# A fused attention, expert and feed-forward kernel: load order at the start, the links of routing, and a first chunk in two banks

## The reference

```
q_bits = (einsum('bhsd,dk->bhsk', q, proj) > 0); same for k
scores = where(q_bucket == k_bucket, scale * q @ k.T, -1e9)
attn   = exp(scores - max) / (sum + 1e-9);  x = attn @ v
```

```
logits = x @ w_gate + modality_bias[modality_id];  e = argmax(logits)
out[e_idx == e] = gate * (relu(x @ w1[e]) @ w2[e])         # 512 -> 1024 -> 512
h = x @ w_in;  g = max(h, 0) + alpha * min(h, 0);  y = g @ w_out   # 512 -> 2048 -> 512
```

## Time and profile before

| | before |
|---|---|
| median of 3 runs | 696.58 us (695.50 to 698.93) |
| profiled execution | 695.9 us, span 694.0 us |
| busy PE, PEld | 684.2, 610.8 us |
| busy DVE, ACT, POOL | 465.9, 353.9, 223.3 us |
| granted TensorE clock | 1.00 |

### The profile page before, as it was taken

How to read it: one execution, slowest core, us unless ns; L and a number is a source line. 1 busy time by engine, 2 the same in 40 slices (tenths; PEclk the granted TensorE clock), 3 DMA queues, 4 the chain that set the end, 5 groups by cost and what they waited for, 6 DMA issues and landing times.

```text
span 694.0 us, 12262 instructions
## 1 busy us (share of the span) xinstructions
PE 684.2 (99%) x4049; PEld 610.8 (88%) x4051; DVE 465.9 (67%) x1017; ACT 353.9 (51%) x692; POOL 223.3 (32%) x320
## 2 busy tenths in 40 slices
PE   7999999999999999999999999999999999999998
PEld 5899999999999998889988998888888888888886
DVE  6998989899999989523511216666676666666664
ACT  5888888888887783114311215333343333433332
POOL 8855465555657960412014200600017000010000
PEclk9999999999999999999999999999999999999999
DMA  6995766749363513870113008200003000010001
GB/s 180 214 263 158 202 206 152 221 117 253 94 168 90 197 40 104 295 248 30 45 60 95 26 31 274 60 0 0 0 16 106 0 0 0 1 60 0 0 1 60
DMA packets 48243, 70.58 MB, mean 102 GB/s; under 512 B 7294, under 2 KB 27470, under 8 KB 48198
## 3 DMA queue, kind: packets, MB, share of 16 engines
q1 hardware_dynamic: 41636, 57.50, 29.0%
q0 software_dynamic: 2832, 8.45, 4.1%
q10 hardware_dynamic: 3730, 4.07, 1.7%
HBM read 33.46 MB, written 17.30 MB: 73 GB/s over the span
## 4 chain that ended last, share of the span: by engine, by line
PE 87%; DVE 6%; ACT 2%; DMA 2%; POOL 1%; issue 1%; SPq 1%; ACTq 0%; DVEq 0%; POOLq 0%
PE bank L1005 7%; PE bank L1232 6%; PE bank L1222 6%; PE bank L1223 6%; PE bank L1233 6%; PE bank L1234 6%; PE bank L1224 6%; PE bank L1024 4%; PE bank L989 4%; PE bank L1026 4%; PE bank L990 4%; PE bank L1167 3%; PE bank L1171 3%; PE bank L1169 3%; PE bank L1130 3%; PE bank L1131 3%
## 5 line engine op out<-in xcount | busy, mean ns | idle before, releaser
L1337 ACT ACTIVATE probs<-bank,raffine 128x768 f32<-128x768 f32 x96 | 95.3, 992 | 28.7 <-DVE raffine L1624 28.4
L1616 DVE TENSOR_REDUCE bank<-bank 128x1 f32<-128x768 f32 x96 | 92.2, 961 | 4.7 <-PE bank L990 3.6
L1005 PE MATMUL bank<-cst,probs 128*128 128x128 f32 x576 | 80.4, 274 | 1.0 <-DVE pt_lo L1632 0.3
L1481 ACT ACTIVATE wi_hi<-ff_raw 128x512 fp32r (+1 forms) x48 | 30.4, 633 | 90.9 <-PE bank L1224 90.8
L1925 DVE SCALAR_TENSOR_TENSOR ht_lo<-bank,ht_hi 128x512 fp32r<-128x512 f32 x28 | 19.0, 689 | 85.4 <-ACT ht_hi L1423 85.4
L1005 PEld LDWEIGHTS bank<-cst,probs 128*128 128x128 f32 x576 | 67.3, 140 | 9.0 <-issue 3.9
L1632 DVE TENSOR_TENSOR pt_lo<-bank,pt_hi 128x384 fp32r<-128x384 f32 x128 | 70.5, 551 | 6.0 <-ACT pt_hi L1354 3.8
L1222 PE MATMUL bank<-x_hi,wi_hi 128*128 128x512 f32 (+1 forms) x192 | 74.5, 388 | 0.0
L1223 PE MATMUL bank<-x_lo,wi_hi 128*128 128x512 f32 (+1 forms) x192 | 73.9, 385 | 0.0
L1224 PE MATMUL bank<-x_hi,wi_lo 128*128 128x512 f32 (+1 forms) x192 | 73.9, 385 | 0.0
L2055 DVE TENSOR_SCALAR neg<-bank,alpha_sb 128x512 f32<-128x512 f32 x47 | 35.3, 751 | 57.4 <-PE bank L1224 57.4
(11 more groups left out here) (316 smaller groups left out, 1625.7 us busy)
## 6 DMA issues: line engine op xcount, KB each, us to landing
stacks<-nat SPq DMA_DIRECT2D x84, 192.0 KB, 4.3
y_slots<-zeros SPq DMA_DIRECT2D x14, 512.0 KB, 5.5
w_raw<-in_moe_w SPq DMA_DIRECT2D x6, 1024.0 KB, 7.6
ff_raw<-in_moe_w_in SPq DMA_DIRECT2D x8, 512.0 KB, 8.8
ff_raw<-in_moe_w_out SPq DMA_DIRECT2D x4, 1024.0 KB, 9.5
y_slots<-y_sb ACTq DMA_DIRECT2D x14, 256.0 KB, 2.0
v_raw<-in_v SPq DMA_DIRECT2D x16, 192.0 KB, 3.7
x_rows<-x_out SPq DMA_DIRECT2D x8, 384.0 KB, 3.0
```

What stands on the lines that cost most here:

```text
L1005: mm = pe.transpose(lane[1 + hf][:, t * P:t * P + P], probs[:, m % 3, kt * P:kt * P + P], C["ident"])
L1337: act.activation(probs[:, m % 3, :].rearrange("p (a c) -> p a c", a=2), s_ps[m % 2], ACT.Exp, bias=raffine[:, col, 1:2], scale=raffine[:, ...
L1616: dve.tensor_reduce(rmin_ps[n % 2], s_ps[n % 2], AX.XY, ALU.min).then_inc(rmin_done, 1)
```

## The change

- SP and ACT queues at the start: ACT issues k's second half first, then the projection, then q's first half of the second head; its other q half goes to SP.
- `WARM` is 14 matmuls instead of 10, and three new ones run between the transposes and the features.
- `first_features("fq", 0, TOP)` goes behind the first `row_scale` on DVE.
- `row_sums` runs on ACT, two steps before the fold, into two buffers of `rden`.
- Routing: the counts are added up by PE over six tiles' one-hots, the first batch's sums and the padding (no reduction on DVE); the shift and the padding are added to the ranks by one more matmul (`extra_b`, made on POOL); the block number comes from a table times 256 (`excl_rows`, POOL) in one product and one sum; the links for the block table move behind the index; `row_hot_b` is made by twelve operations with a scalar per partition instead of one.
- `load_expert(1)` goes behind the wait for the rows of block 1.
- The first chunk's halves go to banks 4 and 6, the second waits for ACT's copy out of bank 6, and DVE makes the activation of each half by itself.
- POOL waits for the second chunk before it gates the second group's tiles.

```diff
-WARM = (10, 12, 9, 3)
+WARM = (14, 12, 9, 3, 3)
...
@@ SP: start, experts
+            sp.dma_start(q_pair[:, HT:QT, 1, :], q_r[1][:, HT:QT]).then_inc(q_first[1], 16)
...
-            with sp.If(n_used > 1):
-                load_expert(1)
             for hf in range(2):
                 sp.wait_ge(w1_ready[hf], 1)
             for tt in range(BT):
                 sp.wait_ge(rows_in[tt], 32)
+            with sp.If(n_used > 1):
+                load_expert(1)
@@ POOL
+            pool.wait_ge(lead_ready, 1)
+            pool.tensor_copy(pad_b[:], pad_e[:]).then_inc(extra_made, 1)
+            pool.tensor_copy(one_hot_b[:, 0:QT], one_hot[:, 0:QT]).then_inc(extra_made, 1)
+            pool.tensor_tensor(extra_b[:], shift[:].unsqueeze(2).broadcast_to([P, TT, E]),
+                               pad_e[:].unsqueeze(1).broadcast_to([P, TT, E]), ALU.add).then_inc(extra_made, 1)
+            pool.tensor_scalar(excl_rows[:], excl_e[:], float(BLOCK), None, ALU.mult).then_inc(extra_made, 1)
...
+                if grp == 1:
+                    pool.wait_ge(g_ready, 2)
@@ PE: start, route_counts, up
+            keep_warm(WARM[4], 3)
             pe.wait_ge(sel_ready, 1)
...
-                pe.wait_ge(part_ready, 1)
-                pe.matmul(cnt_ps, ones_b[:], per_part_b[:], start=True, stop=True).then_inc(count_made, 1)
+                pe.wait_ge(extra_made, 4)
+                pe.wait_ge(norm_done, 2 * BH)
+                pe.matmul(cnt_ps, ones_b[:], part0_b[:], start=True, stop=False)
+                pe.matmul(cnt_ps, ident_b[:], pad_b[:], start=False, stop=False)
                 pe.wait_ge(hot_ready, 1)
+                for c in range(QT, TT):
+                    mm = pe.matmul(cnt_ps, ones_b[:], one_hot_b[:, c], start=False, stop=c == TT - 1)
+                mm.then_inc(count_made, 1)
...
+                pe.matmul(rank_ps, ident_b[:], extra_b[:].rearrange("p t e -> p (t e)"), start=False, stop=True,
+                          skip_group_check=True)
...
+                    if part:
+                        pe.wait_ge(y_out, last_block * BT + 2)
...
+                    if parts > 1:
+                        dst = first_up_ps[part]
...
+                    if part + 1 < parts:
+                        mm.then_inc(half_up, 1)
@@ ACT: start, row sums
-            act.dma_start(proj_raw[:], proj.unsqueeze(0).broadcast_to([2, HD, BITS])).then_inc(proj_in, 16)
             act.dma_start(k_pair[:, :, 1, :], k_r[1]).then_inc(k_first, 16)
-            for hf in range(2):
-                ts = slice(hf * HT, hf * HT + HT)
-                act.dma_start(q_pair[:, ts, 1, :], q_r[1][:, ts]).then_inc(q_first[hf], 16)
+            act.dma_start(proj_raw[:], proj.unsqueeze(0).broadcast_to([2, HD, BITS])).then_inc(proj_in, 16)
+            act.dma_start(q_pair[:, 0:HT, 1, :], q_r[1][:, 0:HT]).then_inc(q_first[0], 16)
...
+                if n % 3 == 0 and n >= 6:
+                    row_sums(n // 3 - 2)
@@ DVE: routing
-            then(dve.tensor_tensor(one_hot[:, second], key[:], six(kmax[:], E), ALU.is_equal))
-            then(dve.tensor_reduce(per_part[:], one_hot[:].rearrange("p t e -> p e t"), AX.X, ALU.add))
-            dve.tensor_copy(per_part_b[:], per_part[:]).then_inc(part_ready, 1)
-            dve.tensor_copy(one_hot_b[:], one_hot[:]).then_inc(hot_ready, 1)
+            dve.tensor_tensor(one_hot_b[:, second], key[:], six(kmax[:], E), ALU.is_equal).then_inc(hot_ready, 1)
...
-            then(dve.tensor_tensor(padded[:], cnt_ps, pad_e[:], ALU.add))
-            slots = go(dve.tensor_tensor(cmp6[:], padded[:].unsqueeze(2).broadcast_to([P, E, JMAX]),
+            slots = go(dve.tensor_tensor(cmp6[:], cnt_ps.unsqueeze(2).broadcast_to([P, E, JMAX]),
                                          row(C["block_start"], E), ALU.is_gt))
...
+            slots = go(dve.tensor_tensor(pair_n[:], row(nblk[:], E), excl_rows[:], ALU.mult))
...
+            slots = go(dve.tensor_reduce(base[:], pair_n[:], AX.X, ALU.add))
...
-            dve.tensor_tensor(row_hot_b[:], tok(srow[:], P), row(iota_b[:], TT), ALU.is_equal
-                              ).then_inc(place_ready, 1)
+            for c in range(TT):
+                last = dve.tensor_scalar(row_hot_b[:, c], iota_b[:], srow[:, c:c + 1], None, ALU.is_equal)
+            last.then_inc(place_ready, 1)
@@ DVE: first chunk
+                    dve.wait_ge(half_up, 1)
+                    dve.tensor_scalar(neg[:, h0], first_up_ps[0], 0.0, alpha_sb[:, 0:1], ALU.min, ALU.mult
+                                      ).then_inc(half_step, 1)
...
+                    dve.scalar_tensor_tensor(act2[:, 0, h0], first_up_ps[0], 0.0, neg[:, h0], ALU.max, ALU.add
+                                             ).then_inc(half_step, 1)
+                    dve.wait_ge(up_made, 1)
...
```

More of the change, by code:

```diff
@@ L286, in build @@
         sort_ps = bank[:, 7, 0:PARTS * QT]
+        first_up_ps = [bank[:, b, 0:GROUP // 2] for b in (4, 6)]
         turn_bank = lambda grp, tt: 6 + tt % 2 if grp else tt
@@ L1355, in turned, with row_sums @@
                                    ).then_inc(pt_hi_done, 1)
+            def row_sums(half):
+                act.wait_ge(exp_done, 3 * half + 3)
+                if half >= 2:
+                    act.wait_ge(norm_step, half - 1)
+                act.activation(rden[:, half % 2], rsum[:, (half // 2) % 2, half % 2 * HT:half % 2 * HT + HT], ACT.Copy,
+                               bias=1e-9).then_inc(rden_made, 1)
             def outputs(half):
@@ L1767, in step @@
                     maxima(n)
-                if half is not None:
-                    row_sums(half)
                 if 0 <= n - 2 < STEPS:
@@ L1859, in _ @@
             after(slots)
-            slots = go(dve.scalar_tensor_tensor(base[:], base[:], float(BLOCK), pad_e[:], ALU.mult, ALU.add))
+            slots = go(dve.tensor_tensor(cmp27[:], tok(pos[:], SLOT_TILES - 1), row(C["tile_start"], TT),
+                                         ALU.is_ge))
             dve.tensor_reduce(table_f[:, TB_NU:TB_NU + 1], used[:], AX.X, ALU.add)
+            after(slots)
+            slots = go(dve.tensor_reduce(stile[:], cmp27[:], AX.X, ALU.add))
             after(experts)
@@ L1905, in _ @@
                               ).then_inc(place_ready, 1)
+            after(experts)
+            dve.tensor_copy(table[:, 0:N_FIRST], table_f[:, 0:N_FIRST]).then_inc(first_ready, 1)
             def split_w1(u, halves=range(2)):
@@ L1937, in _ @@
             hidden(0, range(2, 4))
-            then(dve.tensor_tensor(pair_c[:], row(count0[:], E), excl_e[:], ALU.mult))
+            blocks = go(dve.tensor_tensor(pair_n[:], row(nblk[:], E), incl_e[:], ALU.mult))
+            go(dve.tensor_tensor(pair_c[:], row(count0[:], E), excl_e[:], ALU.mult))
+            after(blocks)
+            blocks = go(dve.tensor_reduce(cum[:], pair_n[:], AX.X, ALU.add))
+            after(links[0] - 1)
             then(dve.tensor_reduce(cbase[:], pair_c[:], AX.X, ALU.add))
@@ L1943, in _ @@
             dve.tensor_copy(slot_s[:, QT:TT], pos[:, QT:TT])
+            nxt = table_f[:, TB_U + 1:TB_U + NBMAX + 1]
+            after(blocks)
+            then(dve.tensor_tensor(leq[:], row(cum[:], NBMAX + 1),
+                                   C["block_no"].unsqueeze(2).broadcast_to([P, NBMAX + 1, E]), ALU.is_le))
+            then(dve.tensor_tensor(leq[:], leq[:], row(used[:], NBMAX + 1), ALU.mult))
+            then(dve.tensor_reduce(table_f[:, TB_U:TB_U + NBMAX + 1], leq[:], AX.X, ALU.add))
+            go(dve.tensor_scalar(swt[:], nxt, table_f[:, TB_NU:TB_NU + 1], None, ALU.is_lt))
+            blocks = go(dve.tensor_tensor(table_f[:, TB_SW:TB_SW + NBMAX], nxt,
+                                          table_f[:, TB_U:TB_U + NBMAX], ALU.subtract))
             dve.wait_ge(gexp_done, 1)
@@ L1975, in _ @@
             dve.wait_ge(rank_read, 1)
+            then(dve.tensor_tensor(posc[:], posc[:], extra_b[:, 0:QT], ALU.subtract))
             then(dve.tensor_tensor(posc[:], posc[:], first_hot, ALU.mult))
@@ L2047, in split_tiles, with chunk @@
                                       ).then_inc(x2_ready, 1)
-            def chunk(grp, f, par, last=False, tiles=()):
+            def chunk(grp, f, par, last=False, tiles=(), first=False):
                 c = f + grp * FC2
@@ L2073, in _ @@
             for grp in range(GROUPS):
-                chunk(grp, 0, 0)
+                chunk(grp, 0, 0, first=grp == 0)
                 if grp:
```

114 lines of the change are left out of this document (53 added, 61 removed).

## The result

The changed kernel takes 693.49 us (median of six, 692.99 to 694.12) where the kernel before took 697.36 beside it (695.5 to 698.93): a ratio of 0.9947, interval 0.9931 to 0.9962. Run twice more it gave 0.9959 (0.9945 to 0.9972) and 0.9954 (0.994 to 0.9967). The forecast was 694.2, "within 0.5%"; the measured gain, 0.41 to 0.53% by the three ratios, lies on that border.

A forecast was written before the change was run, and what follows sets the result against it. PE was taken as the bound, busy 99% of 694.0 us. Start 0.5, attention 0.15, routing 0.9 and first chunk 0.37 gave 1.9 us off 695.9; forecast 694.2, "within 0.5%", range 691.4 to 696.4.

The forecast's parts named there:

- The start: First loads, warming and deferral: k lands earlier and PE's transposes start sooner; gain 0.5 us, bounds -0.2 and 0.9.
- rival 3: At the start: no gain, because q is late or the clock rises late; 694.7 to 695.1, 695.7 with both; chance 0.2.
- Warming, not the load, is last: Before k's transposes: fourteen warming matmuls end after k lands, so transposes start at 6.02 instead of 6.74, gaining 0.72 us.
- The deferral: Ramp on DVE: a feature piece moved behind the first row scale costs 0 to 0.3 us, taken as 0.1.
- Attention: Row sums moved from DVE to ACT close some late PE waits: gain 0.15 us, at best 1.5, at worst 6.4 lost.
- rival 2: In attention: ACT becomes the bound through the added sums, PE waits in all 32 halves; 4.6 us lost, 700.5; chance 0.06.
- rival 1: Late attention waits close too and the start gives its upper bound: 4 us gained, 692.1; chance 0.24.
- Routing: Shorter DVE chain to the index tiles removes PE's wait there: gain 0.9 us, bounds 0.6 and 1.2.
- The part of the chain behind the comparison: Routing on DVE: block-table links moved away save 0.2 us, twelve one-hots at 0.13 replacing one of 1.75 save 0.15.
- The counts: Routing on PE: the 0.25 us wait goes, eight more tiny matmuls cost 0.24; net 0.0, bounds -0.1 and 0.15.
- Weight loads behind the rows: Second expert's loads go behind block 1's gathers and meet block 2's, with 6 us spare: worth nothing unless landing doubles.
- Two banks: Second network's first chunk in halves: DVE ends 0.5 us earlier, PE gains 0.37 at the first down projection.

The follow-up runs named there:

- start alone: Kernel before with new first-load order, 14 plus 3 more warming matmuls and the feature deferral: 695.25 us against 696.55, ratio 0.9985.
- all but the start: Changed kernel with the three edits of its start undone: 694.91 us, ratio 0.998 to the kernel before.
- loads alone: Kernel before with only the first loads reordered (k ahead of the projection, q's second half from SP): 695.14 us against 696.94, ratio 0.9979.
- routing alone: Kernel before with only the new counts, DVE chain and tables: 696.86 us, ratio 1.0001.
- short warming: Changed kernel with ten warming matmuls and none behind the transposes, new loads kept: 692.76 us, ratio 0.9945; repeated 693.15 us, ratio 0.995.
- weights ahead: Changed kernel with the second expert's weights again issued ahead of the waits for the rows: 694.62 us, ratio 0.9971 to the kernel before.

## Why the prediction was right, and where it was not

**The sum.** It said 1.9 off the profiled execution, and 2.5 came; 694.2 against 693.49. The direction and the range held, but not each term. In the pair of profiles the start gave 0.49, attention 0.16, routing 1.20 (0.28 and 0.92), the experts 0.10 and the second network 0.56. That routing's share arrived is luck in one respect: it hung on the moved weight loads, which the prediction priced at nothing.

**The start: the mis-sized term.** The prediction had 0.5, and the pair of profiles has 0.49. The medians have 1.3 to 1.8 (start alone 1.3, all but the start 1.7, loads alone 1.8), the ratios or means 1.0 to 1.5. The step that failed is the one that read the start from one execution of before, as if it were typical. Behind the first scores, the three profiles of before and of kernels with its routing and its DVE sums (before, start alone, loads alone) have 684.40, 684.15 and 684.40 us to the end of the execution (its time less the start of the scores). A median of 696.6 then stands for first scores at about 12.3 us. This is an estimate from the medians; scores as late as that stand in two profiles, at 12.26 and 12.74. The one of before, at 11.50, was on the lucky side: 17 of 59 recorded executions of before took no longer than its 695.9. The prediction did see that its execution was 0.7 below the median of three, and split the difference without asking where the 0.7 lay.

The rule of the Trainium skill that the prediction weighed ("TensorE: Matmul & The Clock Gate", section "What's actually happening": the moment of the rise differs from run to run) was borne out: the same ten warming matmuls took 3.79, 3.97, 4.41 and (in four profiles) 4.45 us. But I charged it only to the new kernel, as rival 3. It was the old one that suffered. With an idle stretch of 1.1 to 1.6 us between the warming and k, it stayed at or fell back to 1.2 GHz in two of three profiles. With k early, none of the eleven profiles did so past the transposes of k. That the order of the loads narrows and lowers the times is shown by the run that changes it alone. That slow starts belong to the old order, and that they explain 0.6 of its 1.5 us, follows from the mean clocks (32 of 80 against 0 of 79), as far as a low mean is a slow start. That it is the idle stretch which brings them is argued from the two slow profiles; no run kept k late and filled the stretch with warming, so that link is not tested by itself.

"Warming, not the load, is last" was right for that execution (transposes at 6.03, forecast 6.02), and without value: the chain runs through q (landed at 6.87) and the projection (5.86, in the bound given), so features came at 8.10, not near 7.8. The deferral cost nothing that shows.

**Attention.** 0.15 forecast, 0.16 in the pair, about 0.3 over fourteen profiles. The late waits went only from 4.5 to 4.3 us, and ACT became no bound: rival 2 fell, and so did the half of rival 1 that lay in attention. The other half of rival 1, a start worth its upper bound of 0.9, is about what the times show (1.0 to 1.8). So its 4 us lie near the 3.9 of the first medians, but not for the reason that made it a rival.

**Routing.** The seven links took 0.273 each (forecast 0.275), the one-hots 0.16 (forecast 0.13), and the index wait went whole: 7.47 to 6.55, 0.92 for 0.91. The part of the chain behind the comparison was mis-sized: 0.35 was to come off and 0.10 did (4.65 to 4.55 us up to the end of the last index tile). The prediction took 1.75, a duration with its tail, as the price of the single one-hot; by the distance of starts it was 1.67, so the twelve cost 0.28 more and not 0.15 less. It cost nothing, as the tiles were done at 273.99 and PE came to them at 274.30: the spare time was 0.31 us, not the 0.6 of the forecast. The counts gave 0.28 where I had 0.0. From the last up matmul to the first counts one it was 0.53 (267.67 to the 268.20 of the earlier trace rows) and is 0.12; the 0.25 in brackets, which I had counted, leaves out the turn from one stage to the next that went with the wait. The eight more matmuls took 0.13 of it, not 0.24.

**Weight loads behind the rows: priced at nothing, worth the whole of the routing.** "Nothing" was read from the transfers of before, where the load was all but over when the gathers began. The failing step is "the table that SP, ACT and PE read for the next block is written after the same number of links as now ... nothing". It was written 1.99 us after the count's first reader, and is now written 6.38 after it. The question was not when PE needs the table but whom else its reader, SP's queue, would meet: 3.5 us later it met the gathers. Without this part the routing would have been worth nothing (1.0001).

**Two banks.** 0.37 forecast, 0.54 measured. The first down projection comes 0.38 sooner after the first up matmul, as forecast. What the term left out stands behind it: before, the next matmul started 0.34 us after that one, now 0.23, another 0.11. The wait for y_sb stayed covered (the copy ends at 423.08, PE starts the second half at 423.88), as the prediction had it.

## What to carry over

A saving taken from one pair of profiles at the very start of a kernel is a draw from a scatter: compare the spread of the times as well as their medians, and the mean granted clock of each execution too. In this kernel the earlier load of k was worth 1.5 us and longer warming nothing that shows, so look first at idle stretches of PE behind the warming and at the load that ends them. When a chain is reordered, follow every reader of what now comes later, DMA queues first, and ask which transfer it will then coincide with. And cut the profiles at the same events: behind the start the stages repeated to 0.1 us, where whole times scattered by 1 to 3.

## Not expected of the hardware

The column of the granted clock does not show every slow stretch. In the profile of all but the start the windows from 8 to 10 us (the second is shown) say 1.00 while its feature matmuls start 0.32 us apart (0.18 at the higher level); in the routing alone the same spacing goes with 0.50:

```profile
9.00:10.00 1.00, 1.00 (x3) 1.00 (x4) 0.92 (x2) 0.97 (x2) 1.00 (x2) 1.00 0.81 257
```

At the start, the durations of matmuls of one shape are the safer clock. And landings scatter. With the same order of loads PE waited 0.16 us for q in the first profile of short warming, 0.52 in its repeat and 0.58 in the one with the weights ahead, though the transposes of q began at 7.06, 6.56 and 7.20; in the third profile of the changed kernel they began at 6.34 with no wait. The landings alone move the scores by some tenths of a microsecond.
